# Transposes of the attention result placed behind the transposes of the probabilities

## The reference

```python
# q, k, v: (4, 8, 768, 64); n_global 8, n_local 96
scores = scale * np.matmul(q, k.transpose(0, 1, 3, 2))
is_global = pos[None, :] < int(n_global)
is_local = (rel >= 0) & (rel < int(n_local))
keep = is_global | is_local
scores = scores + bias[None, :, :, :]          # -slope of the head * distance
scores = np.where(keep, scores, -1000000000.0)
a = np.exp(scores - np.max(scores, axis=-1, keepdims=True))
a = a / (np.sum(a, axis=-1, keepdims=True) + 1e-09)
attn_out = np.matmul(a, v)
x = attn_out.transpose(0, 2, 1, 3).reshape(B * S, H * D)
logits = x @ phi                               # (3072, 32)
d = softmax(logits, over all tokens)
slot_input = d.T @ x                           # 32 slots
slot_out = relu(slot_input @ w1[e]) @ w2[e]    # 8 experts, 4 slots each
x = softmax(logits, over the slots) @ slot_out
out = np.maximum(x @ w_in, 0.0) ** 2 @ w_out
```

## Time and profile before

| | us |
|---|---|
| median of three executions | 514.47 |
| the profiled execution | 514.65 |
| its span, first to last instruction | 512.9 |
| PE busy in the span | 488.4 (95%) |
| PE weight loads | 399.3 (78%) |
| DVE busy | 363.5 (71%) |
| ACT busy | 346.5 (68%) |
| POOL busy | 94.8 (18%) |

### The profile page before, as it was taken

How to read it: one execution, slowest core, us unless ns; L and a number is a source line. 1 busy time by engine, 2 the same in 40 slices (tenths; PEclk the granted TensorE clock), 3 DMA queues, 4 the chain that set the end, 5 groups by cost and what they waited for, 6 DMA issues and landing times.

```text
span 512.9 us, 12775 instructions
## 1 busy us (share of the span) xinstructions
PE 488.4 (95%) x4573; PEld 399.3 (78%) x4573; DVE 363.5 (71%) x1024; ACT 346.5 (68%) x758; POOL 94.8 (18%) x223
## 2 busy tenths in 40 slices
PE   2999999999999998689999999999999999999997
PEld 1767766776666642324789999999999999999996
DVE  6687786787787671305998987787776877858783
ACT  2788887887888610005998977777677777777740
POOL 1455544545445303400000000000000000000000
PEclk9999999999999999799999999999999999999999
DMA  7699889884565699996001011010100101011011
GB/s 288 242 359 360 332 300 326 327 320 140 177 199 173 210 346 411 385 386 245 0 1 43 0 43 42 1 41 0 41 21 20 41 0 41 0 41 41 0 42 42
DMA packets 24587, 77.24 MB, mean 151 GB/s; under 512 B 2400, under 2 KB 2400, under 8 KB 22112
## 3 DMA queue, kind: packets, MB, share of 16 engines
q1 hardware_dynamic: 19536, 60.95, 32.7%
q10 hardware_dynamic: 5008, 15.73, 8.3%
HBM read 70.39 MB, written 6.29 MB: 150 GB/s over the span
## 4 chain that ended last, share of the span: by engine, by line
PE 83%; DVE 6%; ACT 4%; issue 2%; POOL 2%; DMA 1%; ACTq 0%; DVEq 0%; POOLq 0%
PE bank L1551 14%; PE bank L1552 14%; PE bank L1553 14%; PE bank L1232 7%; PE bank L1220 4%; PE bank L1523 4%; PE bank L1247 4%; ACT probs L974 3%; PE bank L1457 3%; PE bank L1477 3%; PE bank L1252 2%; PE bank L1282 2%; POOL probs L435 2%; PE bank L1272 2%; PE bank L1215 2%
## 5 line engine op out<-in xcount | busy, mean ns | idle before, releaser
L974 ACT ACTIVATE probs<-probs,nmax 128x232 f32<-128x232 f32 (+1 forms) x192 | 88.6, 463 | 33.4 <-DVE nmax L525 33.4
L435 POOL TENSOR_SCALAR probs<-probs,rden 128x232 f32<-128x232 f32 (+1 forms) x192 | 82.8, 452 | 91.9 <-DVE rden L534 91.9
L1551 PE MATMUL bank<-t_hi,s_hi 128*128 128x256 f32 x352 | 98.7, 280 | 0.0
L1552 PE MATMUL bank<-t_lo,s_hi 128*128 128x256 f32 x352 | 98.6, 280 | 0.0
L1553 PE MATMUL bank<-t_hi,s_lo 128*128 128x256 f32 x352 | 98.5, 280 | 0.0
L525 DVE CUSTOM_DVE_ANT_0 probs<-bank,bias 128x232 f32<-128x232 f32 (+1 forms) x192 | 61.7, 378 | 25.2 <-PE bank L1220 21.8
L1097 ACT ACTIVATE g_s<-bank 128x1024 f32<-128x1024 f32 x48 | 49.0, 1023 | 30.5 <-PE bank L1523 30.5
L1126 ACT ACTIVATE s_hi<-s 128x512 fp32r<-128x512 f32 x88 | 55.1, 627 | 19.1 <-DVE s L908 14.6
L1551 PEld LDWEIGHTS bank<-t_hi,s_hi 128*128 128x128 f32 x352 | 66.5, 189 | 0.0
L1552 PEld LDWEIGHTS bank<-t_lo,s_hi 128*128 128x128 f32 x352 | 66.4, 189 | 0.0
L1553 PEld LDWEIGHTS bank<-t_hi,s_lo 128*128 128x128 f32 x352 | 66.4, 189 | 0.0
(11 more groups left out here) (189 smaller groups left out, 997.0 us busy)
## 6 DMA issues: line engine op xcount, KB each, us to landing
qkv_s<-qkv_dram SPq DMA_DIRECT2D x15, 1028.0 KB, 7.5
qkv_s<-qkv_dram SPq DMA_DIRECT2D x16, 704.0 KB, 5.0
w_s<-w_dram ACTq DMA_DIRECT2D x5, 2048.0 KB, 9.7
w_s<-w_dram SPq DMA_DIRECT2D x15, 512.0 KB, 8.6
out_dram<-o_stage SPq DMA_DIRECT2D x24, 256.0 KB, 2.0
w_a<-w_dram SPq DMA_DIRECT2D x9, 512.0 KB, 8.2
wo_raw<-w_out_dram SPq DMA_DIRECT2D x4, 1024.0 KB, 13.4
w_pre<-w_dram ACTq DMA_DIRECT2D x1, 2048.0 KB, 13.0
```

What stands on the lines that cost most here:

```text
L435: last = pool.tensor_scalar(probs[:, v % 2, m, a, 0:w], probs[:, v % 2, m, a, 0:w], rden[:, v % 2, m, a:a + 1], 1.0, ALU.mult, ALU.mult)
L974: act.activation(probs[:, v % 2, m, a, 0:w], probs[:, v % 2, m, a, 0:w], ACT.Exp, bias=nmax[:, v % 2, m, a:a + 1], scale=-1.0, accum_out=d ...
L1551: pe.matmul(OUT[n], hi, W_HI[n](at_f), start=(c == 0 and f == 0 and n in (0, 2, 4, 5)), stop=False, skip_group_check=True)
L1552: pe.matmul(OUT[n], hi, W_LO[n](at_f), start=False, stop=False, skip_group_check=True)
```

## The change

`to_tokens` is split. The small products that need `x_t` or `x_nat` of earlier steps (`share`, `dispatch`) become `small_products`, directly behind the scores, for the pair three steps back as before. The result transposes, with `back` behind them for v = 1 and 3, stand at the end of PE's step and belong to the pair two steps back, one step earlier than before. `nat_ready` is raised by whichever comes last for a pair. The slot maxima are taken at the end of step 2 instead of 3. DVE's, ACT's, POOL's and SP's programs are otherwise the same.

```diff
-        MAX_STEP, EXP_STEP = 3, 4
+        MAX_STEP, EXP_STEP = 2, 4
...
+            def small_products(b, v):
+
+                if v % GRP == GRP - 1:
+                    share(v // GRP, [(v - GRP + 1 + g) % 4 for g in range(GRP)]).then_inc(nat_ready, 1)
+                elif b > 0 and v in SLOT_HALF:
+                    n = SLOT_HALF.index(v)
+                    for t in range(2):
+                        last = dispatch(SHARE, TILES * ((b - 1) % 2), t, slice(n * 2 * P, (n + 1) * 2 * P))
+                    last.then_inc(nat_ready, 1)
+
             def to_tokens(b, v):
 
-                p = v // GRP
                 pe.wait_ge(xt_copied, b * STEPS + (1 + v + 1))
                 pe.wait_ge(nat_copied, b * STEPS + (v + 1))
                 for m in range(2):
                     last = pe.transpose(NAT[:, m * P:(m + 1) * P], x_t[:, v % 4, m * P:(m + 1) * P], ident[:, :])
-                if v % GRP == GRP - 1:
-                    last = share(p, [(v - GRP + 1 + g) % 4 for g in range(GRP)])
+                if v % GRP == GRP - 1 or (b > 0 and v in SLOT_HALF):
+                    return
                 if b > 0 and v == LOG_BACK:
                     last = back(SHARE, log_t)
                 elif b > 0 and v == DISP_BACK:
                     pe.wait_ge(disp_exped, b * 2)
                     last = back(SHARE, disp_t)
-                elif b > 0 and v in SLOT_HALF:
-                    n = SLOT_HALF.index(v)
-                    for t in range(2):
-                        last = dispatch(SHARE, TILES * ((b - 1) % 2), t, slice(n * 2 * P, (n + 1) * 2 * P))
                 last.then_inc(nat_ready, 1)
 
             def step(b, s, prev):
@@ -1299,11 +1304,13 @@
                 if s >= 3 or prev:
                     if s == 3 and not prev:
                         pe.wait_ge(phi_in, 16)
-                    to_tokens(*before(b, s, 3))
-                if (s >= 2 or prev) and s < STEPS + 2:
+                    small_products(*before(b, s, 3))
+                if s >= 2 or prev:
                     weigh_values(*before(b, s, 2))
                 if (s >= 1 or prev) and s < STEPS + 1:
                     transpose_probs(*before(b, s, 1))
+                if (s >= 2 or prev) and s < STEPS + 1:
+                    to_tokens(*before(b, s, 2))
```

## The result

The changed kernel takes 527.65 us (median of four executions, 527.02 to 528.37), the kernel before 515.13 us beside it. The ratio is 1.0258 with a 95% interval of 1.0241 to 1.0274: slower by 12.5 us. The forecast was 527.3 us, slower by 12.7.

What follows compares the result with a forecast made beforehand. PE was taken to bound attention; afterwards a PE-DVE loop would set most steps. Batch 0 from step 3 +2.5, its step 2 +0.2, later batches +3.4, +3.4, +3.2: +12.7 on 514.65, so 527.3 us; range 520.5 to 531.5.

Steps and rivals of the forecast that it cites:

- The bound before: Attention stage of the kernel before: PE sets the step, 2.94, 3.57 or 3.29 us, with no wait for another engine.
- The loop: Each attention step: scores, bias, token copy, x_t copy, result transposes, scores; 3.51, 3.83, 3.43 or 3.76 us.
- the pair and its boundary: Two result transposes plus the change of form to the scores on PE: taken as 0.37 us, ends 0.21 and 0.44.
- Step 7: Step 7 of batches 1 to 3: 3.83 us, every extra DVE operation taken at 0.32 us like the addition.
- Steps 4 and 6: Steps 4 and 6 of batches 1 to 3: 3.83 and 3.76 us, extra DVE operations at 0.32 us each.
- Step 5: Step 5 of batches 1 to 3, with a share and back of the weights: 4.09 us.
- Step 3: Step 3 of batches 1 to 3, with back of the logits: 3.69 us, slot maxima costed at nothing.
- The slot maxima: Four small DVE operations moved one step forward: costed at nothing, at most 0.3 us in three places, 0.9.
- PE stays the bound and the saved boundary counts: Rival for the attention stage: one boundary less per step gains 7 us, 507.6 us; chance 5%.
- the two cancel: Rival: saved boundary and new wait balance, 514 to 516 us, needing a loop of about 3.49 us; chance 4%.
- waits add up: Rival: POOL's late scaling and the slot maxima add to the loop instead of being covered, 531 us; chance 8%.
- The clock: Granted clock in attention expected to stay 1.00; rival that it falls for one batch, past 560 us, chance 1%.

Runs made afterwards that it cites:

- the short scaling: POOL scaling only 32 of 232 columns: 511.81 us on the kernel before, 526.02 us on the changed kernel.
- Experiments 1 to 3: Changed kernel with x_t copy ahead of token copy, 532.37 us; transposes reading an older x_t, 517.76; extra DVE operation, 541.19 (in the kernel before, 515.25).
- experiment 7: Kernel before with result transposes directly ahead of the probability transposes, still for the pair three steps back, x_t copied before tokens: 512.70 us against 514.43.
- experiment 5: POOL scaling 32 of 232 columns: changed kernel 526.02 us, kernel before 511.81, changed kernel with transposes reading an older x_t 515.70.
- experiment 1: Changed kernel with DVE's x_t copy ahead of the token copy instead of behind it: 532.37 us, ratio 1.0356.

## Why the prediction was right

- **The bound before**, PE from start to start, held: the extra operation on DVE cost that kernel 0.7 us in 48 steps. It was not quite as free as I wrote ("Nothing in them waits for another engine"): the short scaling took 3 us off it.
- **The loop** held in each of its terms: 1.05 us to the bias, 0.06 from the end of the `x_t` copy to PE, 0.36 to 0.37 to the scores. The value I had taken for the pair and its boundary, between 0.21 and 0.44, was the one measured. Experiments 1 to 3 show by intervention that it is this loop: another order, a wait less, an operation more.
- **The steps.** Forecast and measured for a batch, from the starts of the scores in batch 2:

| step | 0 | 1 | 2 | 3 | 4 | 5 | 6 | 7 | 8 | 9 | 10 | 11 |
|---|---|---|---|---|---|---|---|---|---|---|---|---|
| forecast | 3.43 | 3.51 | 3.83 | 3.69 | 3.83 | 4.09 | 3.76 | 3.83 | 3.83 | 4.12 | 3.51 | 3.83 |
| measured | 3.43 | 3.50 | 3.83 | 3.79 | 3.77 | 4.00 | 3.69 | 4.03 | 3.83 | 4.13 | 3.50 | 3.83 |

- **Where terms were off.** Step 7: I let the addition of the slots cost 0.32 us; with the small operation for the sums ahead of it (L596) it holds the `x_t` copy back by 0.52. Steps 4 and 6: the copies of the logits and weights cost less than 0.32, some 0.26. Step 5: `back` behind the result transposes has their form, and the two together cost 0.53, not 0.37 + 0.26. Step 3: the slot maxima were not free. These cancel within 0.1 us a batch, which is luck as much as merit.
- **The slot maxima** delay the bias of step 3 by 0.2 us (1.39 instead of 1.19 after the scores), inside the 0.3 that was the bound, three times 0.2 in all. Timeline of DVE:

```profile
107.81 0.42 DVE L584 TENSOR_REDUCE small<-log_t 96x1 f32<-96x256 f32 x1
108.26 0.27 DVE L586 SCALAR_TENSOR_TENSOR small<-small 96x1 f32<-96x1 f32 x1
108.57 0.40 DVE L588 TENSOR_TENSOR small<-small 96x1 f32<-96x1 f32 x1
109.00 0.15 DVE L590 COPY small<-small 96x1 f32<-96x1 f32 x1
109.19 0.29 DVE L525 CUSTOM_DVE_ANT_0 probs<-bank,bias 128x128 f32<-128x128 f32 x1
```

- **The sum by batches**: 2.5, 3.4, 3.4, 3.2 forecast, 2.2, 3.5, 3.5, 3.3 measured. In batch 0 six of the nine steps came out at 3.38, 3.46 and 3.79 us, 0.04 shorter each than the same steps later. The difference is in the first term, from the scores to the bias, 1.14 and 1.01 us there instead of 1.19 and 1.05; why is open.
- **Waits**: 21.0 us before the result transposes, "some 20" forecast, with 0.50 us in a plain step and 0.27 in one with a share. Clock, DVE's 1.05 us and the stages after attention as forecast, but for the clock's 0.9 us in one execution.
- **The rivals.** That PE stays the bound and the saved boundary counts (507.6 us) falls for this kernel, though its price per step is real: the step with a dispatch and first tiles, where PE is the longer path, came down from 4.28 to 4.13 us. The rule of the Trainium skill's page "TensorEngine Tiling (Array Packing)", Key Properties, that a change of tiling mode drains TensorE, agrees with the trace in so far as each boundary costs 0.16 us; that a drain is what costs it, no run shows. But the rival's 7 us are not there even without the loop: experiment 7 has the same boundary saved and no new wait on DVE, and gains 1.7. That ACT and POOL follow closely behind PE and take the rest is argued from its timelines, not tried. I had reckoned only with PE and this one loop. That the two cancel (514 to 516) falls with the time. That waits add up (531 us) falls: POOL shortened, the changed kernel gained 1.6 us in the medians and 0.6 in the steps of its trace. The clock did not fall: it stayed at 1.00 in attention, though PE was not busy for 3.3 of each 45.4 us.

## What to carry to other kernels

On an engine in program order, ask of each moved step not only what it costs but how old its input is at the new place: when this work moved a step nearer to its producer, a wait that had always been met became a round trip PE, DVE, PE in each step, and a saving of 0.16 us a step became a loss of 0.3. Write the round trip down as a sum from the row where it starts to the row where it closes; an engine that is busy 70% can still set the pace by its order. And to save a boundary, look for a neighbour of the same form that doesn't need younger data: ahead of the probability transposes the same two transposes won 0.4%.

## What the runs showed of the hardware

- Some of DVE's small operations on SBUF get longer beside POOL's scaling. L586 and L588, on 96x1 elements, take 0.27 and 0.40 us in the timeline above, where POOL scales blocks of 128x232 from 108.07 to 109.83; in the kernel before, where it scales blocks of 128x128, they take 0.18 and 0.31. With the short scaling, blocks of 128x32 from 107.52 to 108.60, the same two, one line further down, take:

```profile
107.71 0.15 DVE L587 SCALAR_TENSOR_TENSOR small<-small 96x1 f32<-96x1 f32 x1
107.90 0.18 DVE L589 TENSOR_TENSOR small<-small 96x1 f32<-96x1 f32 x1
```

  In all three L586 starts 0.19 us behind the start of the scaling, so the times go with the width of POOL's blocks and not with POOL working at all. The copy L590, between the same small columns, takes 0.15 us in all three, and the large DVE operations that read a PSUM bank (0.40 to 0.42 us) show no such difference. That fits experiment 5, where the slot maxima no longer delay step 3: from the start of L584 to the end of L590 it is 1.34 us in the changed kernel and 1.00 with the short scaling.
- From the end of the operation that releases them to the result transposes it takes 0.06 us behind the `x_t` copy (138.13 to 138.19) and 0.14 behind the token copy (97.47 to 97.61). It isn't what the token copy writes: in experiment 1 the time is 0.14 to 0.15 us as well where the addition to `log_t`, the copy of the logits or the addition of the slots raises `nat_copied` last. What makes the difference between the two semaphores was not tried.
- Executions of the changed kernel differed by 1.3 us with the granted clock: 527.02 us at a mean of 0.994, 528.3 at 0.990.
